# An attention and MLP kernel on one core: GpSimd takes over the split of one probability tile in three, the sign projections move one unit earlier, and the first MLP tiles are begun and activated while the last heads are still worked on

## The chip, the core and the metric

The kernel runs on one core of one Trainium2 chip. TensorE (PE in the rows) multiplies matrices into PSUM; ScalarE (ACT), VectorE (DVE) and GpSimd (POOL) work elementwise, GpSimd on SBUF alone; SyncE (SP) issues most transfers. The engines run side by side, each through its own instructions in order, and wait for one another by semaphores. The metric is the device time of a launch in microseconds.

## The reference

Attention over 2 batches of 8 heads, 768 tokens, head size 64, with a mask by hash bucket, then two MLPs over 1536 tokens with model size 512 and hidden size 2048.

```python
q_bits = (einsum('bhsd,dk->bhsk', q, proj) > 0)      # 6 bits: the bucket of a token
k_bits = (einsum('bhsd,dk->bhsk', k, proj) > 0)
mask = q_bucket[:, :, :, None] == k_bucket[:, :, None, :]
scores = where(mask, scale * q @ k.T, -1e9)
attn = exp(scores - max(scores)); attn = attn / (sum(attn) + 1e-9)
x = (attn @ v)                                        # 1536 x 512 over both batches
h = x @ w1_in;  x = where(h > 0, h, exp(min(h, 0)) - 1) @ w1_out
h = x @ w2_in;  out = (s * max(h, 0)**2 + b) @ w2_out
```

## The kernel before

Each product is made in the PE's reduced float format from a high part and a low part: every operand is split into `hi` (rounded) and `lo` (the rest), and a product takes the three terms hi·hi, hi·lo and lo·hi, or two where one side's parts are stacked.

**The heads.** Sixteen heads run as eight pairs. A pair is 12 units of 128 queries, six for each head; three units are a group (`HT = 3`), so a pair has four. Unit k runs on all engines with code written out by hand:

- PE (`unit`, L508 on): the scores of unit k+2 (four matmuls of 384 columns into `s_ps`, L440 and L441), the six transposes of the probabilities of unit k (L448), and then, by the place of k in its group: in the first unit the turn of a finished group (`turn`, L471), in the second and third one half each of the group's product with V (`times_v`, L461 and L462, six matmuls). The projection for the signs of the next head (`project`, L416 to L422, six matmuls) follows in units 1 and 7, the transposes of x (`transpose_x`, L429) in units 4 and 5. These two share the PSUM bank `prep_ps`.
- DVE (`unit`, L738 on): `keep_scores` of unit k+2 (L721), which frees `s_ps` for the next scores; in units 2, 3, 8 and 9 two `write_bits` (L714), one behind `keep_scores` and one behind `split_lo`; `split_lo` of unit k (L728); in the last unit of a group `invert` (L734, L736).
- ACT: the exponential of unit k+1 (L600), `keep_pv` and three copies that normalise a group, and `split_hi` of unit k; all its copies have line L595.
- GpSimd: the splits of q and k (L316 to L322), of V (L340, L342), of x (L329, L331) and of one weight tile in each pair (L349, L351).

The scores of a new head (made in units 4 and 10) need the bits of that head: three of the four `write_bits`. Scores n need `keep_scores` n-1.

**The MLP.** Each of two layers takes three chunks of 512 tokens, each chunk 16 hidden tiles: `hidden(f)` makes one in PSUM (L487, 12 matmuls of 512 columns), ACT applies two functions (L682, L685), DVE makes the result `g` (L802), its high part (L808) and its low part (L810), and `output(f)` multiplies it by the second weight (L505, 12 matmuls). There are four banks for hidden tiles (`HBANKS`) and three buffers for a split result (`GRING`). `hidden(f)` waits until L802 of tile f-4 has read its bank (`h_free`); L808 of tile j waits until `output(j-3)` has read its buffer (`g_free`). DVE takes L802, L808, L810 of one tile after another, in order. Output runs two tiles behind hidden. Chunk 0 of layer 1 needs the heads of batch 0 only, so `hidden(0)` to `hidden(3)` stand between the last units of the last pair. Weight tiles 0 to 7 (`wa`) are split during the heads, 8 to 15 (`wb`) after the last transpose of x, because one of the raw weight buffers holds x until then.

```python
pe.wait_ge(h_free, step + 1)                      # hidden: 4 given at the start, 1 by each L802
dve.wait_ge(g_free, step + 1)                     # L807: 3 given at the start, 1 by each output
nc.vector.tensor_copy(hi[:], g[:]).then_inc(g_made, 1)
```

## Time and profile before

| what | us |
|---|---|
| median of 3 runs (lowest, highest) | 846.91 (846.63, 848.03) |
| the profiled execution: its time, its span | 847.2, 845.4 |
| PE, DVE, ACT, POOL busy over the span | 94%, 51%, 40%, 26% |
| the heads, up to the first hidden tile | 0 to 304.6 |
| the rest of the heads with hidden tiles 0 to 3 | 304.6 to 328.8 |
| from the first output tile to the end | 328.8 to 845.4 |

The busy share is a mean over stages with different limits. In the page's 40 slices (21 us each) PE stands at 6 to 9 tenths over the heads, DVE at 7 and 8, and PE at 9 tenths in every slice from the seventeenth on but the last. The granted clock of PE is 6 tenths in the first slice, 8 in the second and 9 (90% or more) in all after it but the sixteenth. The time of a row is its start from the start of the span, then its duration; matmul rows overlap, since the end of one is modelled with its drain, so how long a step occupies PE is read from start to start. What stands in brackets is the idle time of the engine before the row and what ended it.

### The profile page before, as it was taken

To read this page: it belongs to the slowest core of one execution; us is meant where nothing else is said; L and a number is where in the kernel's file an instruction comes from. 1 tells how busy PE (TensorE), PEld (TensorE's weight loads), DVE (VectorE), ACT (ScalarE), POOL (GpSimd) and SP (SyncE) were. 2 spreads that over 40 slices of the span, in tenths; PEclk is the share of its full clock that TensorE was granted. 3 is DMA by queue.
4 is the path that set the end of the run, shared out by engine and by line. 5 is a ranking of instruction groups with operands and counts; after the bars stand their busy time and mean duration, and the time that the engine had idled before them with its cause. 6 is when DMAs were issued, how large, how long until landed. Compare 5 with 4: busy or idle time off the path is not lost.

```text
span 845.4 us, 11759 instructions
## 1 busy us (share of the span) xinstructions
PE 794.2 (94%) x3996; PEld 690.2 (82%) x3996; DVE 432.0 (51%) x734; ACT 337.2 (40%) x643; POOL 216.2 (26%) x182
## 2 busy tenths in 40 slices
PE   6798889889888997999999999999999999999998
PEld 5788888888788886888888888888888888888886
DVE  4788787878877845633433343334223433333223
ACT  4567676766767653222322232223222222212221
POOL 4226353452635124910000006666000000000000
PEclk6899999999999998999999999999999999999999
DMA  4333343233334102410000003222000100010001
GB/s 120 91 76 91 77 119 105 65 90 74 92 79 112 35 1 75 130 45 1 1 1 1 0 0 99 92 90 67 1 1 0 50 0 0 0 50 0 0 0 50
DMA packets 33255, 41.84 MB, mean 49 GB/s; under 512 B 3024, under 2 KB 21584, under 8 KB 33232
## 3 DMA queue, kind: packets, MB, share of 16 engines
q1 hardware_dynamic: 33008, 41.23, 17.3%
q10 hardware_dynamic: 224, 0.30, 0.2%
q8 instruction: 15, 0.25, 0.1%
q14 instruction: 8, 0.07, 0.0%
HBM read 26.58 MB, written 3.15 MB: 35 GB/s over the span
## 4 chain that ended last, share of the span: by engine, by line
PE 85%; DVE 7%; issue 5%; ACT 2%; DMA 0%; DVEq 0%; POOL 0%; SPq 0%; ACTq 0%
PE acc L505 31%; PE h_ps L487 31%; PE pt_ps L448 5%; PE s_ps L440 4%; PE pv_ps L461 3%; PE pv_ps L462 3%; PE s_ps L441 3%; DVE kt L714 2%; DVE pt_lo L728 1%; DVE probs L721 1%; DVE qt L714 1%; PE pv_ps L471 1%; ACT probs L600 1%; PE prep_ps L429 1%; PE prep_ps L422 1%
## 5 line engine op out<-in xcount | busy, mean ns | idle before, releaser
L682 ACT ACTIVATE r_sb<-h_ps 128x512 f32<-128x512 f32 x96 | 57.4, 598 | 359.0 <-PE h_ps L487 359.0
L728 DVE TENSOR_TENSOR pt_lo<-pt_ps,pt_hi 128x768 fp32r<-128x768 f32 x96 | 92.0, 958 | 39.2 <-ACT pt_hi L595 37.6
L804 DVE TENSOR_SCALAR g_sb<-e_sb,sb_scale 128x512 f32<-128x512 f32 x48 | 27.8, 578 | 158.3 <-ACT e_sb L685 158.3
L802 DVE SCALAR_TENSOR_TENSOR g_sb<-e_sb,h_ps 128x512 f32<-128x512 f32 x48 | 33.0, 687 | 147.3 <-ACT e_sb L685 147.3
L595 ACT ACTIVATE pt_hi<-pt_ps 128x768 fp32r<-128x768 f32 x96 | 77.9, 812 | 75.6 <-PE pt_ps L448 75.3
L721 DVE TENSOR_SCALAR_CACHE_REDUCE probs<-s_ps 128x768 f32<-128x768 f32 x96 | 91.9, 958 | 29.2 <-PE s_ps L441 26.0
L440 PE MATMUL s_ps<-kt,qt 128*128 128x384 f32 x192 | 72.3, 376 | 36.2 <-DVE qt L714 31.3
L600 ACT ACTIVATE probs<-probs,row_min 128x768 f32<-128x768 f32 x96 | 89.7, 934 | 11.3 <-DVE probs L721 11.1
L448 PE MATMUL pt_ps<-cst,probs 128*128 128x128 f32 x576 | 82.8, 282 | 0.0
L810 DVE TENSOR_TENSOR g_lo<-g_sb,g_hi 128x512 fp32r<-128x512 f32 x96 | 74.9, 780 | 3.3
L448 PEld LDWEIGHTS pt_ps<-cst,probs 128*128 128x128 f32 x576 | 72.2, 146 | 3.9
L487 PE MATMUL h_ps<-xt_hi,wa_hi 128*128 (+1 forms) x192 | 74.9, 390 | 0.1
L487 PE MATMUL h_ps<-xt_hi,wa_lo 128*128 (+1 forms) x192 | 74.8, 390 | 0.0
L487 PE MATMUL h_ps<-xt_hi,wb_lo 128*128 (+1 forms) x192 | 74.8, 389 | 0.0
L487 PE MATMUL h_ps<-xt_lo,wa_hi 128*128 (+1 forms) x192 | 74.8, 389 | 0.0
L487 PE MATMUL h_ps<-xt_lo,wb_hi 128*128 (+1 forms) x192 | 74.7, 389 | 0.0
L487 PE MATMUL h_ps<-xt_hi,wb_hi 128*128 (+1 forms) x192 | 74.7, 389 | 0.0
L461 PE MATMUL pv_ps<-pt_hi,v_nat 128*128 128x384 f32 x192 | 74.0, 386 | 0.0
L440 PEld LDWEIGHTS s_ps<-kt,qt 128*128 128x128 f32 x192 | 38.2, 199 | 41.8 <-DVE probs L721 28.0
L462 PE MATMUL pv_ps<-pt_lo,v_nat 128*128 128x384 f32 x192 | 67.9, 353 | 0.0
L441 PE MATMUL s_ps<-kt,qt 128*128 128x384 f32 x192 | 67.1, 349 | 0.0
L685 ACT ACTIVATE e_sb<-r_sb 128x512 f32<-128x512 f32 x96 | 60.7, 632 | 10.6
(87 smaller groups left out, 1538.8 us busy)
## 6 DMA issues: line engine op xcount, KB each, us to landing
qt<-kt SPq DMA_DIRECT2D x45, 192.0 KB, 2.7
w_raw<-w_in_dram SPq DMA_DIRECT2D x32, 256.0 KB, 2.8
w_raw<-w_out_dram SPq DMA_DIRECT2D x32, 256.0 KB, 2.9
raw<-qk_dram SPq DMA_DIRECT2D x15, 384.0 KB, 3.3
raw_v<-v_dram SPq DMA_DIRECT2D x16, 192.0 KB, 2.4
out_dram<-o_sb SPq DMA_DIRECT2D x12, 256.0 KB, 2.1
...
```

Of the source, the lines that this page charges most:

```text
L440: mm(s_ps[:, n, 0:HALF], q1, kt1[par][:, cols], start=True, stop=False)
L441: last = mm(s_ps[:, n, 0:HALF], q2, kt2[par][:, cols], start=False, stop=True)
L448: last = nc.tensor.transpose(pt_ps[k % 2][:, r * P:(r + 1) * P], probs[k % SRING][:, r * P:(r + 1) * P], ident)
L461: mm(pv_ps[:, 0:HALF], v_nat[par][:, kt, :], pt_hi[buf][:, kt, :], start=kt == 0, stop=False)
L462: last = mm(pv_ps[:, 0:HALF], v_nat[par][:, kt, :], pt_lo[buf][:, kt, :], start=False, stop=kt == TILES - 1)
L487: last = mm(bank[:], w[a][:, kt * P:(kt + 1) * P], x[b], start=n == 0, stop=n == 3 * KT - 1)
L505: last = mm(acc[n][:], lhs, rhs, start=f == 0 and j == 0, stop=f == FT - 1 and j == 2)
L595: return nc.scalar.activation(dst, src, ACT.Copy, scale=scale)
L600: nc.scalar.activation(probs[k % SRING][:], probs[k % SRING][:], ACT.Exp, bias=row_min[:, k:k + 1], scale=-1.0, accum_out=row_sum[:, k:k + ...
L721: ts(probs[k % SRING][:].rearrange("p (n c) -> p n c", n=2), s_ps[:, :, 0:HALF], CEILING, HUGE, ALU.min, ALU.min, accum_out=row_min[:, k:k ...
L728: tt(pt_lo[(k // HT) % 2][where], pt_ps[k % 2][:, 0:SEQ].rearrange("p (t c) -> p t c", t=TILES), pt_hi[(k // HT) % 2][where].bitcast(F32), ...
L810: tt(lo[:], g[:], hi[:].bitcast(F32), ALU.subtract).then_inc(g_ready, 1)
```

## The change

The rows of the order below name the instructions as the two programs list them, with the line of each program's own text.

The projection for the signs moves from units 1 and 7 to units 0 and 6, and the bits from units 2, 3, 8 and 9 to 1, 2, 7 and 8. On PE, in units 6 and 7 of a pair, before:

```order
L448 MATMUL pt_ps0<-cst,probs0 128x128 x6
L469 REGISTER_ALU
L471 MATMUL pv_ps<-cst,pv_sb 128x64 x3
L521 REGISTER_ALU
L83 REGISTER_ALU
L440 MATMUL s_ps<-kt1_1,qt1_1 128x384
L441 MATMUL s_ps<-kt2_1,qt2_1 128x384
L440 MATMUL s_ps<-kt1_1,qt1_1 128x384
L441 MATMUL s_ps<-kt2_1,qt2_1 128x384
L448 MATMUL pt_ps1<-cst,probs1 128x128 x6
```

and in the changed program:

```order
L474 MATMUL pt_ps0<-cst,probs0 128x128 x6
L498 MATMUL pv_ps<-cst,pv_sb 128x64 x3
L431 REGISTER_ALU
L436 MATMUL prep_ps<-kt1_0,planes_hi 128x384
L437 MATMUL prep_ps<-kt1_0,planes_lo 128x384
L436 MATMUL prep_ps<-kt1_0,planes_hi 128x384
L437 MATMUL prep_ps<-kt1_0,planes_lo 128x384
L442 MATMUL prep_ps<-kt2_0,planes_hi 128x384 x2
L548 REGISTER_ALU
L84 REGISTER_ALU
L460 MATMUL s_ps<-kt1_1,qt1_1 128x384
L461 MATMUL s_ps<-kt2_1,qt2_1 128x384
```

The six matmuls into `prep_ps` now stand behind the turn of unit 6 and ahead of the scores that unit 7 makes; before they stood behind that unit's product with V.

On DVE, units 6 to 8 in the changed program: L758 is `keep_scores`, L782 the normalising multiplication, L789 the low part of x, L751 `write_bits`, L765 `split_lo`:

```order
L789 TENSOR_TENSOR xt_lo<-prep_ps,xt_hi 128x384
L756 REGISTER_ALU
L758 TENSOR_SCALAR probs2,row_min<-s_ps 128x768
L84 REGISTER_ALU
L782 TENSOR_TENSOR w_raw1<-pv_ps,row_inv 128x3x64
L756 REGISTER_ALU
L758 TENSOR_SCALAR probs0,row_min<-s_ps 128x768
L740 REGISTER_ALU
L745 REGISTER_ALU
L751 TENSOR_SCALAR kt2_0<-prep_ps,cst 12x384
L763 ISA
L765 TENSOR_TENSOR pt_lo0<-pt_ps1,pt_hi0 128x6x128
```

Before, the first unit of a group had its `split_lo` too, and the normalising copies and x's high part were ACT's. Now GpSimd makes both parts of that tile (`split_pt`) from a copy that ACT writes to SBUF, and DVE normalises and makes the low part of x straight from PSUM.

On PE in chunk 0 of layer 1, at the place where bank `h_ps0` is taken by hidden tile 8 (the first with `wb`), before:

```order
L505 MATMUL acc3<-g_hi2,wa_hi 128x512
L505 MATMUL acc3<-g_lo2,wa_hi 128x512
L505 MATMUL acc3<-g_hi2,wa_lo 128x512
L487 MATMUL h_ps0<-xt_hi,wb_hi 128x512
L487 MATMUL h_ps0<-xt_lo,wb_hi 128x512
L487 MATMUL h_ps0<-xt_hi,wb_lo 128x512
```

and in the changed program:

```order
L532 MATMUL acc3<-g_hi0,wa_hi 128x512
L532 MATMUL acc3<-g_lo0,wa_hi 128x512
L532 MATMUL acc3<-g_hi0,wa_lo 128x512
L514 MATMUL h_ps0<-xt_hi,wb_hi 128x512
L514 MATMUL h_ps0<-xt_lo,wb_hi 128x512
L514 MATMUL h_ps0<-xt_hi,wb_lo 128x512
```

Before, output tile 5 (the sixth, in ring buffer 2) stood ahead of hidden tile 8; now it is output tile 0. The seven hidden tiles 0 to 6 are all made among the last steps of the heads, and outputs run seven tiles behind.

The diff, cut to what the prediction speaks of (the planes of signs are also loaded in a compact form of 48 columns and laid out by DVE; with that and the matmuls of `keep_warm` the start changes):

```diff
--- before.py
+++ after.py
-WARM = 12
+WARM, REWARM = 14, 5
 HBANKS, GRING = 4, 3
+BEGUN = HBANKS + GRING
...
-Z_UNIT = {1: 1, TILES + 1: 2}
-BITS_UNIT = {2: (1, (0, 1)), 3: (1, (2, 3)), TILES + 2: (2, (0, 1)), TILES + 3: (2, (2, 3))}
-X_UNIT = {4: 0, 5: 1}
+Z_UNIT = {0: 1, TILES: 2}
+BITS_UNIT = {1: (1, (0, 1)), 2: (1, (2, 3)), TILES + 1: (2, (0, 1)), TILES + 2: (2, (2, 3))}
+X_UNIT = {3: 0, 5: 1}
+X_LO_UNIT = {4: 0, 6: 1}
+W_PAIRS = EARLY // 2
...
 sync: pair
-                load_w(0, i, 0, i)
+                if w:
+                    load_w(0, i + 1, 0, i + 1)
...
 gpsimd
-            def split_x(i, n):
...
+            def split_pt(i, g):
+                G, buf = GROUPS * i + g, g % 2
+                pool.wait_ge(pt_kept, G + 1)
+                pool.nop(nofuse=True)
+                src = pt_raw[buf][:].rearrange("p (t c) -> p t c", t=TILES)
+                nc.gpsimd.tensor_copy(pt_hi[buf][:, :, 0:P], src).then_inc(pt_pool_hi, 1)
+                pool.wait_ge(pt_pool_hi, G + 1)
+                nc.gpsimd.tensor_tensor(pt_lo[buf][:, :, 0:P], src, pt_hi[buf][:, :, 0:P].bitcast(F32),
+                                        ALU.subtract).then_inc(pt_pool_done, 1)
...
-            def pair(i, first=False, more=True):
+            def pair(i, w=True, more=True):
+                split_pt(i, 0)
+                if w:
+                    split_w(at(wa_hi, i), at(wa_lo, i), i, 0, i + 1)
                 split_v(2 * i + 1, 1)
                 if more:
                     split_qk(2 * i + 2, 0)
-                if not first:
-                    split_x(i - 1, 0)
-                    split_x(i - 1, 1)
-                split_w(at(wa_hi, i), at(wa_lo, i), i, 0, i + 1)
+                split_pt(i, 1)
+                split_pt(i, 2)
                 if more:
                     split_v(2 * i + 2, 0)
                     split_qk(2 * i + 3, 1)
+                split_pt(i, 3)
...
 tensor: transpose_probs, times_v
-                wait(pe, pt_lo_done, u - 1)
+                G, t = GROUPS * i + (k - 2) // HT, (k - 2) % HT
+                if t == 0:
+                    wait(pe, pt_kept, G + 1)
+                else:
+                    wait(pe, pt_lo_done, 2 * G + t)
...
-                        pe.wait_ge(pt_lo_done, HT * G + HT)
+                        pe.wait_ge(pt_pool_done, G + 1)
+                        pe.wait_ge(pt_lo_done, 2 * G + 2)
...
 tensor: the start
-            for _ in range(WARM):
-                mm(pv_ps[:, 0:HALF], pt_hi[0][:, 0, 0:P], pt_hi[0][:, 0, :], start=True, stop=True)
+            keep_warm(WARM)
             project(0, 0)
+            keep_warm(REWARM)
...
             for k in range(AHEAD):
                 scores(k, k)
+                keep_warm(REWARM - 2)
...
 tensor: the end of the heads
             hidden(0, 0, 2)
             turn(PAIRS, -2)
             hidden(0, 0, 3)
             times_v(PAIRS, -1, range(TILES))
-            pe.wait_ge(x_kept, 2 * PAIRS - 2)
             transpose_x(PAIRS, 0)
+            hidden(0, 0, 4)
             turn(PAIRS, -1)
-            pe.wait_ge(x_kept, 2 * PAIRS - 1)
+            hidden(0, 0, 5)
+            pe.wait_ge(xt_lo_done, 2 * PAIRS - 1)
             transpose_x(PAIRS, 1)
-            def chunk(layer, c, begun=0):
+            hidden(0, 0, 6)
+            def chunk(layer, c, lead=2):
                 if layer:
                     pe.wait_ge(acc_free, KT * c + 2 * KT)
-                for f in range(FT + 1):
-                    if begun <= f < FT:
+                for f in range(FT + lead):
+                    if f < FT and (lead == 2 or f >= lead):
                         hidden(layer, c, f)
-                    if f >= 2:
-                        output(layer, c, f - 2)
-                output(layer, c, FT - 1)
-            chunk(0, 0, HBANKS)
+                    if f >= lead:
+                        output(layer, c, f - lead)
+            chunk(0, 0, BEGUN)
...
 scalar
+                if t == 0:
+                    wait(act, pt_pool_done, G - 1)
+                    copy(pt_raw[(k // HT) % 2][:], src).then_inc(pt_kept, 1)
+                else:
+                    copy(pt_hi[(k // HT) % 2][:, :, t * P:(t + 1) * P],
+                         src.rearrange("p (t c) -> p t c", t=TILES)).then_inc(pt_hi_done, 1)
...
-            def normalise(i, g):
...
-                copy(x_raw[n][:], prep_ps[:, 0:HALF]).then_inc(x_kept, 1)
+                copy(xt_hi[:, x_cols(i, n)], prep_ps[:, 0:HALF]).then_inc(xt_hi_done, 1)
...
 scalar: the end of the heads
+            activate(0, 0, 0)
             keep_pv(PAIRS, -2)
-            normalise(PAIRS, -2)
+            activate(0, 0, 1)
+            activate(0, 0, 2)
             keep_pv(PAIRS, -1)
-            keep_x(PAIRS - 1, 0)
-            normalise(PAIRS, -1)
-            keep_x(PAIRS - 1, 1)
+            x_hi(PAIRS - 1, 0)
+            activate(0, 0, 3)
+            x_hi(PAIRS - 1, 1)
+            for f in range(HBANKS, FT):
+                activate(0, 0, f)
...
 vector
+            def normalise(i, g):
...
+                tt(x_nat[:, (g % 2) * HT:(g % 2 + 1) * HT, par * DH:(par + 1) * DH],
+                   pv_ps[:, 0:HT * DH].rearrange("p (t d) -> p t d", t=HT),
+                   row_inv[:, c].unsqueeze(2).to_broadcast([P, HT, DH]), ALU.mult).then_inc(x_done, 1)
+            def x_lo(i, n):
+                dve.wait_ge(xt_hi_done, 2 * i + n + 1)
+                cols = x_cols(i, n)
+                tt(xt_lo[:, cols], prep_ps[:, 0:HALF], xt_hi[:, cols].bitcast(F32), ALU.subtract).then_inc(xt_lo_done, 1)
...
 vector: unit
+                if third == 1 and not (first and k < 2 * HT):
+                    normalise(i, k // HT - 2)
+                if k in X_LO_UNIT and not first:
+                    x_lo(i - 1, X_LO_UNIT[k])
                 if k < UNITS - AHEAD or more:
                     keep_scores(u + AHEAD, (k + AHEAD) % UNITS)
...
-                split_lo(u, k)
+                if third:
+                    split_lo(i, k)
...
 vector: the end of the heads (split_g holds the three operations of lines 802 to 810 with their waits)
-            dve.wait_ge(x_kept, 2 * PAIRS)
+            split_g(0, 0, 0)
+            normalise(PAIRS, -2)
+            split_g(0, 0, 1)
+            split_g(0, 0, 2)
+            x_lo(PAIRS - 1, 0)
+            normalise(PAIRS, -1)
+            x_lo(PAIRS - 1, 1)
+            dve.wait_ge(xt_lo_done, 2 * PAIRS)
             dve.nop().then_inc(acc_free, KT)
+            for f in range(GRING, FT):
+                split_g(0, 0, f)
```

## Rows read from the trace of the kernel before

**Rows 1.** Windows of core 0: busy time of each engine, then PEclk, DMA share, GB/s

```profile
100.84:136.59 35.75, 31.40 (x212) 30.00 (x211) 29.10 (x53) 25.91 (x55) 16.40 (x17) 1.00 0.36 92
136.59:173.91 37.32, 32.98 (x212) 31.51 (x211) 29.09 (x53) 25.91 (x55) 16.39 (x16) 0.95 0.34 88
```

**Rows 2.** Waits of the whole run: us in total, times, longest

```profile
PE s_ps L440 <- DVE qt L714: 31.3, 16, 4.3
```

**Rows 3.** Timeline of PE in one pair: start, duration, instruction, idle before

```profile
149.40 0.88 PE L471 MATMUL pv_ps<-cst,pv_sb 128*128 128x64 f32 x6 [0.51 <-ACT pv_sb L595]
150.09 0.42 PE L440 MATMUL s_ps<-kt,qt 128*128 128x384 f32 x1
...
153.65 0.34 PE L440 MATMUL s_ps<-kt,qt 128*128 128x384 f32 x1
...
156.07 0.34 PE L440 MATMUL s_ps<-kt,qt 128*128 128x384 f32 x1
...
157.42 0.83 PE L471 MATMUL pv_ps<-cst,pv_sb 128*128 128x64 f32 x6
159.99 0.44 PE L440 MATMUL s_ps<-kt,qt 128*128 128x384 f32 x1 [1.74 <-DVE qt L714]
```

**Rows 4.** Timeline of DVE in the same pair, units 8 and 9

```profile
154.55 0.96 DVE L721 TENSOR_SCALAR_CACHE_REDUCE probs<-s_ps 128x768 f32<-128x768 f32 x1 [0.76 <-PE s_ps L441]
...
156.20 0.96 DVE L728 TENSOR_TENSOR pt_lo<-pt_ps,pt_hi 128x768 fp32r<-128x768 f32 x1
...
157.84 0.16 DVE L734 SCALAR_TENSOR_TENSOR row_inv<-row_sum,cst 128x3 f32<-128x3 f32 x1
...
158.25 0.96 DVE L721 TENSOR_SCALAR_CACHE_REDUCE probs<-s_ps 128x768 f32<-128x768 f32 x1
```

**Rows 5.** Timeline of PE at both ends of the heads and at the first outputs

```profile
16.48 0.66 PE L440 MATMUL s_ps<-kt,qt 128*128 128x384 f32 x1 [1.15 <-DVE probs L721]
...
55.03 0.34 PE L440 MATMUL s_ps<-kt,qt 128*128 128x384 f32 x1
...
276.71 0.34 PE L440 MATMUL s_ps<-kt,qt 128*128 128x384 f32 x1
...
304.60 0.47 PE L487 MATMUL h_ps<-xt_hi,wa_hi 128*128 128x512 f32 x1
...
324.53 0.52 PE L429 MATMUL prep_ps<-cst,w_raw 128*128 128x128 f32 x3 [0.96 <-ACT w_raw L595]
328.77 0.80 PE L505 MATMUL acc<-g_hi,wa_hi 128*128 128x512 f32 x1 [3.72 <-DVE g_lo L810]
...
336.01 0.39 PE L487 MATMUL h_ps<-xt_hi,wa_hi 128*128 128x512 f32 x1
```

**Rows 6.** Timeline of DVE at the first results g

```profile
327.56 0.43 DVE L808 CAST g_hi<-g_sb 128x512 fp32r<-128x512 f32 x1
...
328.63 0.68 DVE L802 SCALAR_TENSOR_TENSOR g_sb<-e_sb,h_ps 128x512 f32<-128x512 f32 x1
...
331.12 0.55 DVE L808 CAST g_hi<-g_sb 128x512 fp32r<-128x512 f32 x1
331.71 2.78 DVE L810 TENSOR_TENSOR g_lo<-g_sb,g_hi 128x512 fp32r<-128x512 f32 x1
...
357.35 0.43 DVE L808 CAST g_hi<-g_sb 128x512 fp32r<-128x512 f32 x1
357.81 1.41 DVE L810 TENSOR_TENSOR g_lo<-g_sb,g_hi 128x512 fp32r<-128x512 f32 x1
```

**Rows 7.** Timeline of POOL, first split of a `wb` tile and last

```profile
330.24 1.15 POOL L349 CAST wb_hi<-w_raw 128x1024 f32 x1 [2.96 <-DMA w_raw<-w_out_dram]
...
358.84 2.64 POOL L351 TENSOR_TENSOR wb_lo<-w_raw,wb_hi 128x1024 f32 x1 [0.16 <-POOL wb_hi L349]
```

**Rows 8.** Group by line, POOL over the heads: count, busy us, mean ns, idle before

```profile
L322 POOL TENSOR_TENSOR kt<-raw,kt 128x768 fp32r<-128x768 f32 x15 | 27.5, 1830 | 1.3
```

**Rows 9.** Timeline of DVE in the first pair, `invert`

```profile
27.09 1.60 DVE L734 SCALAR_TENSOR_TENSOR row_inv<-row_sum,cst 128x3 f32<-128x3 f32 x1
```

More of the change, by code:

```diff
@@ L9 @@
 F32R = mybir.dt.float32r
-BF16 = mybir.dt.bfloat16
 ACT = mybir.ActivationFunctionType
@@ L66, in laid_planes @@
 def laid_planes(proj):
[L69 to L76 removed]
+    c = np.zeros((P, 2, 2, 2, BITS), np.float32)
+    for side, rows in ((0, slice(DH, P)), (1, slice(0, DH))):
+        for n, sign in ((0, -1), (1, 1)):
+            c[rows, 0, side, n] = proj
+            c[rows, 1, side, n] = sign
+    return c.reshape(P, 8 * BITS)
 def wait(eng, sem, value):
@@ L282, in _ @@
             pair(0)
-            with sp.Fori(1, PAIRS - 2) as i:
+            with sp.Fori(1, W_PAIRS) as i:
                 pair(i)
-            pair(PAIRS - 2, after=False)
-            pair(PAIRS - 1, nxt=False, after=False)
+            with sp.Fori(W_PAIRS, PAIRS - 2) as i:
+                pair(i, w=False)
+            pair(PAIRS - 2, w=False, after=False)
+            pair(PAIRS - 1, w=False, nxt=False, after=False)
+            for f in range(W_PAIRS + 1, EARLY):
+                load_w(0, f, 0, f)
             sp.wait_ge(xt_pe, 2 * PAIRS)
@@ L632, in unit @@
                 first = isinstance(i, int) and i == 0
-                if third == 1 and not (first and k < 2 * HT):
-                    normalise(i, k // HT - 2)
                 if k < UNITS - 1 or more:
@@ new lines, in next_hi @@
+            def next_hi(c):
+                for n in range(KT):
+                    if n < KT - 1:
+                        act.wait_ge(acc_done, c * (KT - 1) + n + 1)
+                    else:
+                        act.wait_ge(g_free, c * FT + GRING + FT)
+                    cols = n * TOKENS + c * CHUNK if isinstance(c, int) else None
+                    where = slice(cols, cols + CHUNK) if isinstance(c, int) else bass.ds(c * CHUNK + n * TOKENS, CHUNK)
+                    copy(xt_hi[:, where], acc[n][:]).then_inc(acc_hi_done, 1)
@@ L696, in _ @@
+            x_hi(PAIRS - 1, 0)
[3 more added lines that the diff above has]
+                activate(0, 0, f)
+            next_hi(0)
+            with act.Fori(1, CHUNKS) as c:
+                for f in range(FT):
+                    activate(0, c, f)
+                next_hi(c)
+            with act.Fori(0, CHUNKS) as c:
+                for f in range(FT):
+                    activate(1, c, f)
         @block.vector
@@ L777, in _ @@
             dve.wait_ge(consts_in, 16)
-            for block in range(4):
+            for block in (2, 0, 1, 3):
                 write_bits(0, 0, block)
@@ L826, in x_cols @@
+            with dve.Fori(0, CHUNKS) as c:
+                for f in range(FT):
+                    split_g(1, c, f)
+                keep_output(c)
 def x_cols(i, n):
```

231 lines of the change are left out of this document (114 added, 117 removed).

## The prediction

> **What bounds the kernel now.** I read the windows first, then the waits, then the timeline of PE beside that of DVE. The MLP (from 328.8 us on) is bound by PE, whose matmuls stand back to back there, so it can lose time and not win any. What can be won lies in the heads and at their end. A pair of heads takes 35.75 us where PE keeps its full clock and 37.32 us where the granted clock averages 0.95 [rows 1]; the mean of pairs 1 to 6 is (276.71 - 55.03) / 6 = 36.95 us [rows 5]. The waits give the cause: PE sat idle 31.3 us in 16 waits for the sign bits that DVE writes [rows 2], one in each half of a pair, 1.74 us each [rows 3]. At the end of the heads PE idles again: 3.72 us before the first output, for `g_lo` [rows 5].
>
> PE's own work in a pair: a unit with a product takes 156.07 - 153.65 = 2.42, unit 7 with its projection 153.65 - 150.09 = 3.56, so the projection is 1.06 (0.08 of the rest is a first matmul); scores and transposes of a unit with a turn take 157.42 - 156.07 = 1.35 and the turn 150.09 - 149.40 = 0.69 [rows 3]. Sum: 8 x 2.42 + 4 x 2.04 + 2 x 1.06 + 0.9 for the transposes of x and first matmuls = 30.5. The other 5.2 of the 35.75 are waits.
>
> **The heads, step by step.** DVE in units 8 and 9: `keep_scores` and a `write_bits` together 156.20 - 154.55 = 1.65, `split_lo` and the next `write_bits` 157.84 - 156.20 = 1.64, `invert` 0.41, a `keep_scores` alone 0.96 + 0.08 = 1.04 [rows 4].
> - Removed from DVE: four `split_lo` in a pair, 4 x 0.99 = 4.0. Added: four multiplications of 192 columns and two subtractions of 384. Between nothing and the 0.96 of a full tile each [rows 4]; by columns I take 0.4 and 0.6, so 2.8. DVE does 1.2 less in a pair.
> - The projection moves ahead of the scores of the next unit. This removes the wait for bits (they are written five products earlier than needed) but not the queue on DVE: `keep_scores` of that unit now waits until PE has done the projection and the scores, though bits could be written meanwhile. From there DVE has, in order, two times (1.65 + 1.64), `invert`, `keep_scores`: 6.58 + 0.41 + 1.04 = 8.0. Scores of the next head need that last `keep_scores`.
>   In the second half of a pair: scores of unit 7 start at 0, are read from 0.9, DVE is through at 8.9 to 9.0. PE has 2.42 + 2.42 + 2.04 = 6.9 until it wants them. So 2.1 is waited. In the first half the transposes of x (0.3) move into this stretch: 1.8. A third wait, for `pv_sb` in unit 6 (0.51 before [rows 3]), becomes 0.7, as ACT has x ahead of it.
>   A pair at full clock: 30.5 + 2.1 + 1.8 + 0.7 = 35.1, against 35.75.
> - Three copies of ACT for each group go (ACT's 25.9 of 35.75 us [rows 1]): they bounded nothing.
> - GpSimd has 16.4 busy in a pair [rows 1]. The splits of probabilities add at most two operations of 1.83 [rows 8] four times, 14.6; x's splits and half of the weight tiles go. It stays under 31 of 35. Queued behind a split are those of V, q and k: the split of group 0 is done about 5 us into the pair, V's follows its product (end of unit 2), q and k of the next head end near 14, their projection comes at 17. Products with V want group g's part four units after it was kept, some 10 us, and it is there in 3 to 7. Hidden; uncovered, each us late would cost one.
> - The clock falls after such waits in part of the cases: (36.95 - 35.75) = 1.2 a pair. The new waits are as long, so I leave 1.3. Pairs 1 to 6: 36.4 instead of 36.95, gain 3 (from 0, if DVE's chain is 0.5 longer, to 11, if no clock is lost). Pair 7 up to the first hidden tile: 27.9 before [rows 5], 27.1 by the same count: 0.8.
> - The start: pair 0 takes 55.03 - 16.48 = 38.6 [rows 5]; with its projection a unit earlier it should take what others do, less the products it lacks: 34.5, gain 4. The first scores come earlier through smaller planes and the extra matmuls keep the clock: 3, between 0 and 4.
> Heads together: 11 less, bounds 3 and 20.
>
> **The end of the heads.** From the first hidden tile to hidden tile 4 before: 336.01 - 304.60 = 31.4 [rows 5], for 4 hidden and 2 output tiles (6 x 2.72), two units' transposes and products (3.4), two turns, one whole product (2.1), two transposes of x (0.6), together 23.9. So 7.5 are waits and half clock (1.8 of it: the two outputs from 328.77 took 7.24 instead of 5.44). The change fills all of that: by the order of the diff hidden tiles 4, 5 and 6 stand where PE waited, and their banks are read in time (result 0 about 8 us before hidden tile 4 wants its bank, result 3 about 0.6 us before hidden tile 7 does). Gain 7.5.
>
> But it adds a wait that stands in no row. With outputs seven tiles behind, PE comes to hidden(f), f = 8 to 15, having just finished output(f-8). Its bank is freed by L802 of tile f-4. Behind it on DVE in order is nothing, ahead of it stands L808 of tile f-5, which waits for a buffer that output(f-8) frees. So each time PE finishes an output, DVE must do L808 and L810 of one tile and L802 of the next, before PE may go on; nothing else is queued on PE. Cost of one: signal 0.2, L808 and L810 328.63 - 327.56 = 1.07, L802 0.68, signal 0.06: 2.0 [rows 6]. While GpSimd splits weight tiles, L808 and L810 take longer: six pairs, from 331.12 (3.4 with the wait in L810) to 357.35 (1.87), mean 3.0 [rows 6]; a wait is then 3.9. GpSimd splits from 330.24 to 361.48, that is from 5.7 after the last transpose begins, for 31 us [rows 5, 7]. In the changed order (0 is the start of hidden tile 2) that is 21 to 52, and the waits begin at 23, 33, 42, 52: four at 3.9, four at 2.0, 23.6 in all.
> The clock: after 3.72 idle it cost 1.8, so 4 x 1.8 = 7.2; after 1.74 idle twice in a pair 1.2, so 0.6 for each of the other four, 2.4. Together 33. Lower bound 8 x 2.0 = 16, upper 8 x 3.9 + 8 x 1.8 = 46. Less the 7.5: the end costs 25.5 more, bounds 8.5 and 38.
>
> From output tile 8 on nothing differs. Sum: 847.2 (profiled; the span is 845.4, and 846.9 is the median) - 11 + 25 = 861; I say 860.
>
> **The rivals.**
> - PE becomes the bound of the heads. For it: DVE does 1.2 less, and DVE is the engine waited for. Against: the chain of 8.0 holds neither of the removed `split_lo` at its place. A pair would take 32.5: 6 x 4.4 + 2 + 7 = 35 less, and with the end's 25 more 837. This is the case on the other side; it decides if DVE's chain from the scores of unit 7 is under 6.
> - The waits at the ring are there but bare: no half clock, no blocking. For it: the clock holds through many waits of 1.74. Against: the 3.72. End +8.5, heads -11: 844.5.
> - GpSimd stands in DVE's way in the heads. `invert` has once taken 1.60, when GpSimd's subtraction of k ran [rows 9]; otherwise 0.16 [rows 4]. GpSimd's share of a pair grows from 16 to about 27. With 1.4 more in each of the two chains of a pair, 2.8 x 7 = 20: 880. The Trainium skill (SBUF — State Buffer, Who interferes with whom) says that a DVE instruction with two SBUF inputs is held for the whole of a GpSimd instruction that reads SBUF. The trace agrees with 1.60 in one of 32; by my count of times the chain's `invert` meets the end of a short operation, so I give this little.
> - The change does not do what it says in the heads (the wait for bits stays): then it gains 7, and the end decides: 865, inside the forecast.
>
> **How the numbers follow.** Forecast 0.68 (its own range 850 to 870), PE bound 0.10, bare ring 0.12, GpSimd in the way 0.10. The range 844 to 871 leaves out the first rival, the last and a little of the second's lower side. Under 0.2% (1.7 us) a measurement of this kernel tells nothing: faster 0.10 + 0.08 of the second = 0.18, same 0.06, slower 0.76.
>
> **What would show it.** Right: idle of PE before hidden tiles 8 to 15 of the first chunk, released by L802's successor, eight times 2 to 4 us; no wait for bits; a wait for `keep_scores` in units 4 and 10 of 1 to 2 us; no idle between hidden tile 2 and output 0; the first hidden tile near 293. Wrong: PE back to back in chunk 0, a pair under 34 or over 37.5, or a first hidden tile after 302.

## The result, and the profile after

| | before | after |
|---|---|---|
| median (lowest to highest), us | 847.39 (846.63 to 848.03) | 859.12 (855.59 to 863.72) |
| ratio, 95% interval | | 1.014 (1.009 to 1.019) |
| the profiled execution: its time, its span | 847.2, 845.4 | 863.7, 861.9 |
| first hidden tile | 304.60 | 295.67 |
| from there to the end | 540.8 | 566.2 |

The change makes the kernel slower by 1.4%, as forecast (860). The profiled executions differ by 16.5: the heads give 8.9 back, what follows costs 25.4. The executions of the changed kernel spread over 8 us, those of before over 1.4, and the profiled one is the longest; by the medians the loss is 11.7.

The page of the changed kernel, busy shares and slices (PE 94% before, DVE 51%, ACT 40%, POOL 26%):

```profile
PE 803.1 (93%) x4009; PEld 690.9 (80%) x4009; DVE 416.5 (48%) x752; ACT 318.1 (37%) x547; POOL 274.5 (32%) x214
PE   7888898889998996788999999999999999999998
PEclk9999999999999998799999999999999999999999
```

The shares moved as the edit moved work, from DVE and ACT to GpSimd, and say nothing of the loss. The slices do: PE's slices at 6 and 7 tenths are the sixteenth and seventeenth (323 to 366 us), and there the clock stands at 8 and 7 tenths too.

The waits of the changed kernel, PE as the waiting engine, with DVE's largest wait on PE beside them (us in total, times, longest):

```profile
PE s_ps L460 <- DVE probs L758: 26.9, 33, 2.3
PE h_ps L514 <- DVE g_sb L866: 21.2, 8, 4.1
DVE g_hi L872 <- PE acc L532: 66.0, 13, 8.5
```

The wait for bits [rows 2], 31.3 us in 16, is gone but for one of 1.3 us at the very start. In its place stand two: one for `keep_scores`, and the new one of hidden tiles for their bank. The third line is its mirror: DVE waits for PE as well, though PE waits for DVE. In this stretch each waits for the other in turn.

PE's timeline of the changed kernel, at hidden tile 0 and at the first four hidden tiles that waited (start, duration, instruction, idle before):

```profile
295.67 0.47 PE L514 MATMUL h_ps<-xt_hi,wa_hi 128*128 128x512 f32 x1 [0.49 <-issue]
...
331.96 0.50 PE L514 MATMUL h_ps<-xt_hi,wb_hi 128*128 128x512 f32 x1 [3.86 <-DVE g_sb L866]
...
343.45 0.79 PE L514 MATMUL h_ps<-xt_hi,wb_hi 128*128 128x512 f32 x1 [4.13 <-DVE g_sb L866]
...
354.78 0.79 PE L514 MATMUL h_ps<-xt_hi,wb_hi 128*128 128x512 f32 x1 [4.04 <-DVE g_sb L866]
...
365.01 0.50 PE L514 MATMUL h_ps<-xt_hi,wb_hi 128*128 128x512 f32 x1 [1.84 <-DVE g_sb L866]
```

Hidden tiles 8, 9 and 10 wait some 4 us, 11 to 15 wait 1.84 each: 12.0 + 9.2 = 21.2. The duration 0.79 against 0.50 marks the matmuls that start at half clock behind two of the long waits.

DVE of the changed kernel at the second wait and at the fourth:

```profile
339.35 0.67 DVE L872 CAST g_hi<-g_sb 128x512 fp32r<-128x512 f32 x1 [7.44 <-PE acc L532]
...
363.20 0.43 DVE L872 CAST g_hi<-g_sb 128x512 fp32r<-128x512 f32 x1 [8.47 <-PE acc L532]
363.66 0.69 DVE L874 TENSOR_TENSOR g_lo<-g_sb,g_hi 128x512 fp32r<-128x512 f32 x1
364.27 0.68 DVE L866 SCALAR_TENSOR_TENSOR g_sb<-e_sb,h_ps 128x512 f32<-128x512 f32 x1
```

DVE sits idle 8.47 us until PE has finished an output, then does the cast, the low part and the next result, and releases PE at the end of the third: 364.27 + 0.68 + 0.06 = 365.01. The 0.2 + 1.07 + 0.68 + 0.06 of the forecast is 1.84 here. The cast at 339.35 belongs to the 4.13: there the three take 0.71, 2.66 and 0.68, up to 343.40.

GpSimd of the changed kernel, the second tile it splits in this stretch and the last:

```profile
328.33 2.44 POOL L361 TENSOR_TENSOR wb_lo<-w_raw,wb_hi 128x1024 f32 x1 [0.17 <-POOL wb_hi L359]
...
351.25 2.34 POOL L361 TENSOR_TENSOR wb_lo<-w_raw,wb_hi 128x1024 f32 x1 [0.16 <-POOL wb_hi L359]
```

The last split ends at 353.6. The three long waits end before 355, the five short ones come after it. I had counted the splits to run until 52 us past the start of hidden tile 2 (304.63) and to stretch a fourth wait; they ended at 49.0, and the fourth wait began only at 58.5. I had put the waits some 9.7 apart. They begin 11.2 to 12.4 apart, because the clock lost behind each also pushes the next one back.

The windows, PE, PEld, DVE, ACT and POOL busy us with instructions, then the granted clock: an early pair, a later one at full clock, the one behind it, and the whole stretch from the first hidden tile to the end, of the changed kernel:

```profile
79.75:117.01 37.26, 33.37 (x210) 31.45 (x210) 27.91 (x55) 23.67 (x43) 23.84 (x21) 0.95 0.34 88
154.25:189.47 35.22, 31.77 (x211) 29.84 (x211) 27.52 (x55) 23.66 (x43) 20.55 (x19) 1.00 0.31 78
189.47:226.27 36.80, 33.35 (x210) 31.38 (x211) 27.56 (x55) 23.65 (x43) 20.54 (x19) 0.95 0.30 75
295.67:861.90 566.23, 541.74 (x2358) 445.68 (x2358) 196.10 (x321) 128.00 (x212) 93.55 (x54) 0.98 0.09 30
```

and the same stretch of the kernel before:

```profile
304.60:845.40 540.80, 532.56 (x2358) 441.24 (x2358) 198.63 (x317) 131.42 (x222) 89.14 (x52) 0.99 0.09 29
```

The two stretches hold the same 2358 matmuls, so the rows split the 25.4 exactly: PE idle is 566.23 - 541.74 = 24.5 against 8.2, 16.3 more, and the same matmuls take 541.74 - 532.56 = 9.2 longer, which is the clock.

The pair at full clock takes 35.22, where 35.75 stood [rows 1] and 35.1 was forecast; where GpSimd still splits a weight tile, in the first four pairs, a pair is some 0.4 longer (37.26 against 36.80, both at a mean granted clock of 0.95).

### The profile page after: what moved, and what is told of

Read it like the earlier page. It is cut to its first block, busy times and chain, and to the rows that moved or that the text cites. A ratio compares the mean times of both kernels' runs of the same rounds, so it can differ in the third digit from the quotient of the medians.

```text
span 861.9 us, 11790 instructions
## 1 busy us (share of the span) xinstructions
PE 803.1 (93%) x4009; PEld 690.9 (80%) x4009; DVE 416.5 (48%) x752; ACT 318.1 (37%) x547; POOL 274.5 (32%) x214
## 4 chain that ended last, share of the span: by engine, by line
PE 81%; DVE 11%; issue 5%; ACT 1%; DVEq 0%; DMA 0%; ACTq 0%; SPq 0%
PE h_ps L514 32%; PE acc L532 30%; PE pt_ps L474 4%; PE s_ps L460 3%; PE s_ps L461 3%; PE pv_ps L488 2%; PE pv_ps L489 2%; DVE probs L758 2%; DVE pt_lo L765 2%; DVE kt L751 2%; PE pv_ps L498 2%; DVE qt L751 2%; DVE g_lo L874 1%; PE prep_ps L436 1%; ACT probs L634 1%
## 5 line engine op out<-in xcount | busy, mean ns | idle before, releaser
L758 DVE TENSOR_SCALAR_CACHE_REDUCE probs<-s_ps 128x768 f32<-128x768 f32 x96 | 91.9, 957 | 39.1 <-PE s_ps L461 35.8
L514 PE MATMUL h_ps<-xt_hi,wb_hi 128*128 (+1 forms) x192 | 79.1, 412 | 21.2 <-DVE g_sb L866 21.2
L460 PE MATMUL s_ps<-kt,qt 128*128 128x384 f32 x192 | 69.7, 363 | 28.2 <-DVE probs L758 26.9
L514 PE MATMUL h_ps<-xt_lo,wb_hi 128*128 (+1 forms) x192 | 78.2, 407 | 0.0
L514 PE MATMUL h_ps<-xt_hi,wb_lo 128*128 (+1 forms) x192 | 78.1, 407 | 0.0
L629 ACT ACTIVATE pt_hi<-pt_ps 128x768 fp32r<-128x768 f32 x64 | 52.0, 812 | 66.5 <-PE pt_ps L474 66.5
L872 DVE CAST g_hi<-g_sb 128x512 fp32r<-128x512 f32 x96 | 42.8, 446 | 69.0 <-PE acc L532 66.0
L359 POOL CAST wa_hi<-w_raw 128x1024 f32 (+1 forms) x16 | 17.5, 1094 | 183.8 <-PE acc L532 180.3
L765 DVE TENSOR_TENSOR pt_lo<-pt_ps,pt_hi 128x768 fp32r<-128x768 f32 x64 | 61.3, 958 | 28.3 <-ACT pt_hi L629 27.3
L874 DVE TENSOR_TENSOR g_lo<-g_sb,g_hi 128x512 fp32r<-128x512 f32 x96 | 72.6, 756 | 3.3
```

The lines of the kernel that those rows point to most:

```text
L460: mm(s_ps[:, n, 0:HALF], q1, kt1[par][:, cols], start=True, stop=False)
L514: last = mm(bank[:], w[a][:, kt * P:(kt + 1) * P], x[b], start=n == 0, stop=n == 3 * KT - 1)
L758: ts(probs[k % SRING][:].rearrange("p (n c) -> p n c", n=2), s_ps[:, :, 0:HALF], CEILING, HUGE, ALU.min, ALU.min, accum_out=row_min[:, k:k ...
L765: tt(pt_lo[(k // HT) % 2][where], pt_ps[k % 2][:, 0:SEQ].rearrange("p (t c) -> p t c", t=TILES), pt_hi[(k // HT) % 2][where].bitcast(F32), ...
L874: tt(lo[:], g[:], hi[:].bitcast(F32), ALU.subtract).then_inc(g_ready, 1)
```

## The experiments

Each is a small edit of the changed kernel or of the one before. Ratios are against the kernel before (846.7 to 847.2 in these comparisons).

| experiment | median us | ratio (95%) | first hidden tile | from there to the end |
|---|---|---|---|---|
| outputs six behind | 827.19 | 0.976 (0.974 to 0.978) | 292.56 | 533.5 |
| four buffers for results | 827.66 | 0.977 (0.975 to 0.979) | 292.30 | 533.5 |
| before, outputs seven behind | 875.90 | 1.035 (1.033 to 1.037) | 303.95 | 569.8 |
| weight splits as memsets | 849.37 | 1.004 (1.002 to 1.005) | 289.54 | 557.2 |
| outputs two behind, hidden tiles 4 to 6 not begun early | 830.77 | 0.980 (0.978 to 0.982) | 294.91 | 536.2 |
| before, signs a unit earlier | 842.32 | 0.993 (0.991 to 0.995) | 299.44 | 540.9 |
| six behind, signs at their old units | 831.49 | 0.983 (0.981 to 0.986) | 296.37 | 533.5 |
| six behind, no filler matmuls at the start | 831.18 | 0.981 (0.979 to 0.984) | 295.89 | 533.7 |
| six behind, bits ahead of `keep_scores` | 814.16 | 0.963 (0.961 to 0.965) | 278.32 | 533.5 |
| the same, and `invert` a unit later | 806.19 | 0.952 (0.950 to 0.954) | 271.06 | 533.5 |

### The wait at the ring

My theory: outputs stand seven tiles behind, and seven is the number of PSUM banks (4) plus that of result buffers (3), so at hidden(f) every bank and every buffer is full and PE can go on only through DVE. The rival: with the low part slowed by GpSimd, DVE is simply too slow in this stretch, whatever the depth. One tile less of lead tells them apart, and so does one buffer more.

```diff
-            def chunk(layer, c, lead=2):
+            def chunk(layer, c, lead=2, begun=0):
...
-                    if f < FT and (lead == 2 or f >= lead):
+                    if begun <= f < FT:
...
-            chunk(0, 0, BEGUN)
+            chunk(0, 0, BEGUN - 1, BEGUN)
```

> The changed kernel with one edit: in chunk 0 of layer 1 outputs run six tiles behind hidden tiles, not seven (output 0 stands ahead of hidden tile 7). Ring theory: the buffer that L872 wants is freed a hidden and an output tile (5.4 us) before PE wants the bank, against a chain of 2 to 4 us on DVE, so all eight waits go (21.2 us idle in the profile) and with them the half clock behind them (5 to 12 us): 826 to 831 us, against 859. Rival, the waits come from GpSimd's weight splits and move with them: some of the three waits of 4 us stay, 838 to 845. Rival, PE would only wait for its weight tiles (wb) instead: 840 to 850.

Seven hidden tiles are still begun among the heads, but outputs follow six behind. DVE's timeline with outputs six behind:

```profile
322.33 2.25 DVE L872 CAST g_hi<-g_sb 128x512 fp32r<-128x512 f32 x1 [3.56 <-PE acc L532]
...
350.17 2.79 DVE L874 TENSOR_TENSOR g_lo<-g_sb,g_hi 128x512 fp32r<-128x512 f32 x1
```

and its windows, the first 130 us of the MLP and the whole of it:

```profile
290.00:420.00 130.00, 129.49 (x599) 108.36 (x598) 61.65 (x86) 35.76 (x62) 39.89 (x23) 1.00 0.16 49
292.56:826.10 533.54, 530.22 (x2358) 439.64 (x2358) 200.32 (x321) 128.33 (x212) 94.91 (x54) 1.00 0.10 32
```

DVE's operations are slowed as much as before, up to 2.79 us, and PE doesn't wait once: its idle time in these 130 us is the 0.5 ahead of the first hidden tile. The rival falls. The whole stretch takes 533.5 where the changed kernel takes 566.2: 21.2 less idle and 541.74 - 530.22 = 11.5 less for the same matmuls. This 32.7 is the price of the ring waits with their clock, and I had summed 33.

```diff
-HBANKS, GRING = 4, 3
-BEGUN = HBANKS + GRING
+HBANKS, GRING = 4, 4
+BEGUN = 7
...
-            for f in range(GRING, FT):
+            for f in range(3, FT):
```

> The changed kernel with four buffers for split results in place of three, outputs still seven tiles behind. Ring theory: L872 of tile f-5 then wants output f-9, done 5.4 us before PE comes to hidden tile f, so the eight waits go as with six tiles behind: 826 to 831 us, within 2 us of that kernel. Rival, the order with seven tiles is itself at fault (banks, weights or the late outputs), the ring is not: 850 to 860.

The same from the other side: outputs still seven behind, one more buffer, 827.66. It isn't the depth as such that costs, but depth equal to banks plus buffers.

The converse, the kernel before with outputs of its first chunk seven behind:

```diff
-            def chunk(layer, c, begun=0):
+            def chunk(layer, c, begun=0, lead=2):
...
-                for f in range(FT + 1):
+                for f in range(FT + lead):
...
-                    if f >= 2:
-                        output(layer, c, f - 2)
-                output(layer, c, FT - 1)
+                    if f >= lead:
+                        output(layer, c, f - lead)
...
-            chunk(0, 0, HBANKS)
+            chunk(0, 0, HBANKS, 7)
```

> The kernel before with one edit: hidden tiles 4, 5 and 6 of chunk 0 stand ahead of output 0, and outputs of that chunk run seven tiles behind. Heads and their end are as before. Ring theory: the same eight waits appear and cost 26 to 33 us with the clock; hidden tile 4 still waits for the first result (the 3.7 us stay), nothing is won: 870 to 881 us. Rival, the waits of the changed kernel need its new work on DVE and GpSimd: 845 to 852.

Its PE waits:

```profile
PE s_ps L440 <- DVE qt L713: 31.1, 16, 4.3
PE h_ps L487 <- DVE g_sb L801: 20.8, 9, 3.6
...
326.94 0.79 PE L487 MATMUL h_ps<-xt_hi,wa_hi 128*128 128x512 f32 x1 [2.53 <-DVE g_sb L801]
```

The last line is hidden tile 4, which waits for the first result: 2.53, where output 0 waited 3.72 before. The other eight are hidden tiles 8 to 15 at the ring, 20.8 - 2.5 = 18.2 us (3.6, 3.1 and six of 1.93), in a kernel that has nothing else of the change, and 875.9 - 846.75 = 29.2 us on the median. The heads are as they were (31.1 for bits). So the ring wait needs no other part of the change.

### GpSimd's part in the wait

Three waits are 4.0 and five 1.84. My theory: DVE's two operations on a result are slowed while GpSimd splits weights. The rival: the first three wait for something else of the first tiles, the end of the heads' work on DVE or ACT. In this kernel GpSimd writes the `wb` tiles of the first layer by two memsets, so it reads nothing. The weights of hidden tiles 8 to 15 of that layer are zero here: the kernel leaves their part of layer 1 out. Its loop over these tiles on GpSimd is also written out.

```diff
+            def blank_w(hi, lo, count, buf, landed):
+                pool.wait_ge(w_landed[buf], 32 * landed)
...
+                nc.gpsimd.memset(hi.bitcast(F32), 0.0).then_inc(w_hi, 1)
+                pool.wait_ge(w_hi, count + 1)
+                nc.gpsimd.memset(lo.bitcast(F32), 0.0).then_inc(w_split, 1)
...
-                    split_w(at(wb_hi, 2 * j + n), at(wb_lo, 2 * j + n), EARLY + 2 * j + n, 1 - n,
+                    blank_w(at(wb_hi, 2 * j + n), at(wb_lo, 2 * j + n), EARLY + 2 * j + n, 1 - n,
```

> The changed kernel, with the splits of weight tiles 8 to 15 of layer 1 on GpSimd replaced by two memsets of the same tiles (these weights are zero then, so layer 1 leaves them out). GpSimd then only writes there. Theory that its reads hold up L874 and L872: the three waits of 4 us become 1.8 to 2.0 like the other five, and less clock is lost: 6 us fewer in idle and 1 to 5 in clock, 847 to 853. Rival, writes hold DVE up as well (or another cause, such as the transfers, makes them long): 857 to 861.

The waits of this kernel, and its first wait at the ring:

```profile
PE h_ps L522 <- DVE g_sb L874: 14.7, 8, 1.8
...
323.81 0.50 PE L522 MATMUL h_ps<-xt_hi,wb_hi 128*128 128x512 f32 x1 [1.84 <-DVE g_sb L874]
```

All eight are 1.84, the first three too: 6.5 us less idle. DVE of this kernel beside a memset of GpSimd:

```profile
331.17 0.43 DVE L880 CAST g_hi<-g_sb 128x512 fp32r<-128x512 f32 x1 [7.42 <-PE acc L540]
331.63 0.69 DVE L882 TENSOR_TENSOR g_lo<-g_sb,g_hi 128x512 fp32r<-128x512 f32 x1
```

and GpSimd at the same time:

```profile
331.27 1.22 POOL L367 MEMSET wb_hi<- 128x1024 f32 x1 [0.56 <-DMA w_raw<-w_out_dram]
332.55 0.95 POOL L369 MEMSET wb_lo<- 128x1024 f32 x1
```

The low part takes its bare 0.69 beside a GpSimd instruction that only writes, and 2.7 beside one that reads. The Trainium skill (SBUF — State Buffer, Who interferes with whom) says just this: a DVE instruction with two SBUF inputs collides with a GpSimd instruction that reads SBUF, not with one that only writes it. The trace agrees. It also shows the other direction: the memset that began during DVE's cast took 1.22 instead of 0.95.

The stretch to the end is 9.0 shorter than the changed kernel's (566.2 - 557.2), for 6.5 less idle. Against the 533.5 without ring waits it is 23.7 longer: 14.7 of idle and 9.0 of clock, 1.1 for each short wait. Of the changed kernel's 11.5 of clock that leaves 11.5 - 5 x 1.1 = 6.0 for the three long waits, 2.0 each. These are means: behind a short wait the next one follows after 7.6 us or after 9.2, against 5.44 + 1.84 = 7.3 for two tiles and a wait, so a single one costs 0.3 or 1.9, and the 1.6 between them is what a fall of the clock costs in the heads too.

### What beginning early is worth by itself

Hidden tiles 4 to 6 out of the heads, and outputs two behind as before; what stays is that ACT and DVE turn tiles 0 to 3 into results while the last products run.

```diff
-            hidden(0, 0, 4)
...
-            hidden(0, 0, 5)
...
-            hidden(0, 0, 6)
...
-            chunk(0, 0, BEGUN)
+            chunk(0, 0, 2, HBANKS)
```

> The changed kernel with its depth undone: hidden tiles 0 to 3 begun among the heads and outputs two tiles behind as before, but the early activations on ACT and DVE kept. Theory: without depth there are no ring waits, and since results 0 to 2 are ready early, PE waits at the end of the heads only for the last turn and transpose (up to 2 us, and the 3.7 us before output 0 are gone): 828 to 832, at most 3 us more than with six tiles behind. Rival, depth is what fills the end of the heads: 833 to 836.

PE's waits at the end of the heads in this kernel:

```profile
312.87 0.88 PE L498 MATMUL pv_ps<-cst,pv_sb 128*128 128x64 f32 x6 [0.25 <-ACT pv_sb L626]
...
314.36 0.52 PE L449 MATMUL prep_ps<-cst,w_raw 128*128 128x128 f32 x3 [0.61 <-DVE w_raw L779]
...
316.20 0.47 PE L532 MATMUL acc<-g_hi,wa_hi 128*128 128x512 f32 x1 [1.32 <-DVEq L897]
```

The 3.72 before the first output [rows 5] is down to 1.32, and the 1.32 are no longer for a result: L897 is the instruction by which DVE frees the accumulators behind the last low part of x. The stretch takes 536.2: 4.6 less than before, and 2.7 more than with seven tiles begun and outputs six behind (533.5); on the medians it is 3.6, where I had expected at most 3. Of the 7.5 that I gave to the filling, 4.6 come from the earlier results and 2.7 from tiles 4 to 6; together 7.3.

### The heads: the move, the relief, the start

The kernel before with the signs a unit earlier, and nothing else:

```diff
-Z_UNIT = {1: 1, TILES + 1: 2}
-BITS_UNIT = {2: (1, (0, 1)), 3: (1, (2, 3)), TILES + 2: (2, (0, 1)), TILES + 3: (2, (2, 3))}
+Z_UNIT = {0: 1, TILES: 2}
+BITS_UNIT = {1: (1, (0, 1)), 2: (1, (2, 3)), TILES + 1: (2, (0, 1)), TILES + 2: (2, (2, 3))}
...
-                    if k > TILES and not first:
+                    if k >= TILES and not first:
```

> The kernel before with the move alone: projection in units 0 and 6, bits in units 1, 2, 7 and 8. GpSimd, ACT and DVE keep their work, the end is untouched. Theory of the prediction: the move makes the gain of the heads and DVE's relief makes next to none, as the chain of 8.0 holds none of the removed instructions: pairs near 36.4 and 4 us in pair 0: 838 to 843. Rival, the move is only good with DVE relieved (it has a split_lo in units 0 and 3 as well): 846 to 852.

And the converse, six behind with the signs and x back at their old units, so that of the two edits to the heads only the relief by GpSimd is left (smaller planes and filler matmuls stay, the bits go back to units 2, 3, 8 and 9, and the edit of the lead is the one above):

```diff
-Z_UNIT = {0: 1, TILES: 2}
...
-X_UNIT = {3: 0, 5: 1}
-X_LO_UNIT = {4: 0, 6: 1}
+Z_UNIT = {1: 1, TILES + 1: 2}
...
+X_UNIT = {4: 0, 6: 1}
+X_LO_UNIT = {5: 0, 7: 1}
```

> The changed kernel with outputs six tiles behind (827.2 us), and the projection and bits back in units 1, 7 and 2, 3, 8, 9 (the transposes of x go to units 4 and 6). GpSimd's splits and DVE's relief stay. Theory of the prediction: the wait for bits is back in each half and the relief buys little: pairs of 36.5 to 37.5, pair 0 with its long wait: 831 to 838. Rival, the relief is what shortens the heads: 824 to 829.

The wait for bits in this second kernel:

```profile
PE s_ps L460 <- DVE qt L751: 28.6, 15, 3.2
```

It is back almost in full, with two of three `split_lo` left on DVE. To leave the start out, count from the scores made in unit 10 of pair 0 to the first hidden tile. The windows, in this order: before, relief alone, move alone, both (six behind):

```profile
50.08:304.60 254.52, 225.87 (x1465) 216.63 (x1465) 201.51 (x361) 179.41 (x376) 107.93 (x105) 0.97 0.33 83
42.62:296.37 253.75, 225.07 (x1464) 216.29 (x1465) 191.08 (x375) 164.12 (x295) 154.21 (x130) 0.97 0.31 77
51.26:299.44 248.18, 222.75 (x1464) 210.61 (x1465) 200.37 (x360) 182.47 (x375) 108.04 (x105) 0.99 0.33 85
44.01:292.56 248.55, 224.31 (x1465) 211.32 (x1465) 191.13 (x374) 165.56 (x295) 153.87 (x130) 0.99 0.31 79
```

In the changed kernel's own trace the stretch takes 295.67 - 44.14 = 251.5. Here the relief brings 0.7 and the move 6.3. But only half of the 6.3 is waiting: PE idles 28.65 before and 25.43 with the move, and the other half is that the same matmuls take less. Of the seven parts of this stretch (six pairs and the rest) the clock fell in five before, in five with the relief alone, in two with the move alone, in two with both and in four in the changed kernel. Three falls fewer at 1.6 are 4.8 of the 6.3, which leaves the move 1.5 by itself, some 0.2 in a pair (35.38 to 35.45 at full clock, where 35.44 and 35.74 stood). How many pairs are met differs between executions too, so the move's share is surer from the medians: 846.74 - 842.32 = 4.4 by itself, 831.49 - 827.19 = 4.3 on top of the relief. What is shown is that the move shortens PE's waits (1.74 us become 1.44) and that the clock then falls less often, and that taking work from DVE does next to nothing in this stretch. That DVE's order is what bounds a pair follows from the last two experiments below.

Ahead of this stretch it is the other way round. The move alone reaches the scores of unit 10 at 51.26 against 50.08 before, and with the relief at 44.01 against 42.62 without the move. In pair 0 the wait for bits of 4.34 us in unit 4 only turns into one of 3.59 for `keep_scores`.

The start, six behind without the filler matmuls that keep the clock:

```diff
-WARM, REWARM = 14, 5
+WARM = 12
...
-            keep_warm(REWARM)
...
-                keep_warm(REWARM - 2)
```

> The changed kernel with outputs six tiles behind (827.2 us), without the matmuls of keep_warm behind the first projection and the first scores, and with 12 at the start as before. Theory: PE falls to half clock in the first 20 us as before, which makes scores and transposes of the first units longer; of the 3 us taken for the start about 2 are the clock's: 828 to 832. Rival, the first units are bound by DVE and ACT whatever the clock: 826 to 828.

Its window from 10 to 20 us:

```profile
10.00:20.00 10.00, 7.79 (x27) 6.71 (x26) 2.89 (x6) 3.79 (x7) 4.57 (x5) 0.52 0.56 152
```

and with them (six behind):

```profile
10.00:20.00 10.00, 8.16 (x49) 6.98 (x48) 5.78 (x12) 5.73 (x11) 7.12 (x6) 1.00 0.69 177
```

In the same 10 us PE is about as busy, but at a granted clock of 0.52 it gets 27 matmuls done and at 1.00 it gets 49, of which 6 are filler. The scores made in unit 4 come at 28.84 and at 25.33: the filler is worth 3.5 us at the start, 3.3 at the first hidden tile and 4.0 on the median.

### Shortening the chain of 8.0

The forecast says that the pair is bound by what DVE does between the scores of one unit and the `keep_scores` two units on, and that bits could be written while `keep_scores` waits. If that is right, the same instructions in another order must be faster. First, both blocks of bits of units 1 and 7 go ahead of `keep_scores`:

```diff
+                if blocks and third == 1:
+                    write_bits(2 * i + off, off % 2, blocks[0])
+                    write_bits(2 * i + off, off % 2, blocks[1])
+                    blocks = ()
```

> The changed kernel with outputs six tiles behind (827.2 us) and one more edit: in units 1 and 7 DVE writes both blocks of bits ahead of keep_scores, in the time in which it waits for the projection and the scores of that unit. Chain theory: two blocks (1.3) start 0.7 before the scores can be read, so the chain from there to the keep_scores that PE wants shrinks by about 0.7 in each half of a pair, 15 times 0.7 = 10 us, and up to 5 of clock: 812 to 818. Rival, the wait of PE in units 4 and 10 has another cause than DVE's order (the transposes, ACT): 825 to 829. Rival, keep_scores comes later and delays the exponential and with it the transposes: slower than 829.

Then `invert` also moves behind the next unit's `keep_scores`:

```diff
-                if third == 2:
-                    invert(i, k // HT)
+                if third == 0 and not (first and k == 0):
+                    invert(i, k // HT - 1)
+                if not more and k == UNITS - 1:
+                    invert(i, GROUPS - 1)
```

> The kernel with bits first, and invert of a group moved behind the keep_scores of the next unit, so that the 0.4 us (and what GpSimd adds to it) leave the chain. Chain theory: another 15 x 0.4 = 6 us off: 805 to 813, and PE waits under 0.5 us in units 4 and 10. Rival, once the chain is short PE is bound by its own matmuls and by the wait for pv_sb in unit 6: within 2 us of the kernel with bits first.

PE's waits with bits ahead alone, in units 4 and 10:

```profile
126.88 0.45 PE L460 MATMUL s_ps<-kt,qt 128*128 128x384 f32 x1 [0.80 <-DVE probs L758]
...
144.42 0.45 PE L460 MATMUL s_ps<-kt,qt 128*128 128x384 f32 x1 [1.01 <-DVE probs L758]
```

PE's waits in units 10 and 4 of the last kernel, and the window of a pair:

```profile
140.56 0.44 PE L460 MATMUL s_ps<-kt,qt 128*128 128x384 f32 x1 [0.60 <-DVE probs L758]
...
156.64 0.44 PE L460 MATMUL s_ps<-kt,qt 128*128 128x384 f32 x1 [0.37 <-DVE probs L758]
...
123.43:156.64 33.21, 31.56 (x211) 29.77 (x211) 27.39 (x55) 23.46 (x43) 20.74 (x19) 1.00 0.39 99
```

DVE is as busy as in a pair of the changed kernel (27.39 against 27.52), PE too (31.56 and 31.77), and the pair takes 33.21 instead of 35.22 at the same full clock. The wait in unit 10 goes from 1.44 over 1.01 to 0.60, that in unit 4 from 1.27 (0.85 in the later pairs) over 0.80 to 0.37. I had expected both under 0.5. The granted clock is 1.00 over the whole run in all four executions of this kernel. With bits ahead alone it is 1.00 in two of the four, the profiled one among them, and 0.998 and 0.994 in the others, which took 814.65 and 816.74 us.

This version, 806.19 us (805.41 to 806.38), beats both kernels: 4.8% under the kernel before, 6% under the changed one.

## Why the prediction was right

- **The ring.** Forecast: hidden tiles 8 to 15 wait for the result of tile f-4, 4 x 3.9 + 4 x 2.0 = 23.6. Measured: 12.0 + 5 x 1.84 = 21.2. The mechanism is shown from both sides (six behind, a fourth buffer) and in the kernel before. Mis-sized: three waits met GpSimd's splits where four were counted. The splits ended 3 us sooner and the waits stand further apart (11.2 to 12.4 us, not 9.7); either would have spared the fourth.
- **The clock behind it.** Forecast 9.6 (1.8 behind a long wait, 0.6 behind a short one), measured 11.5 (2.0 and 1.1). The 0.6 came from waits that stand twice in a pair; these follow each other after 7.6 to 9.2 us. That the sum is right, 32.7 against 33, is partly luck: the wait was put 2.4 too high and its clock 1.9 too low.
- **What is filled.** Forecast 7.5, measured 540.8 - 533.5 = 7.3. No idle of PE stood between hidden tile 2 and output 0.
- **The pair.** Forecast 35.1 at full clock, measured 35.22 (35.61 in a pair with a weight split). The chain of 8.0, in units 7 to 10 of the changed kernel's DVE:

```profile
146.18 0.96 DVE L758 TENSOR_SCALAR_CACHE_REDUCE probs<-s_ps 128x768 f32<-128x768 f32 x1 [1.30 <-PE s_ps L461]
...
152.74 0.24 DVE L771 SCALAR_TENSOR_TENSOR row_inv<-row_sum,cst 128x3 f32<-128x3 f32 x1
153.23 0.96 DVE L758 TENSOR_SCALAR_CACHE_REDUCE probs<-s_ps 128x768 f32<-128x768 f32 x1
```

and PE at its end:

```profile
154.25 0.44 PE L460 MATMUL s_ps<-kt,qt 128*128 128x384 f32 x1 [1.44 <-DVE probs L758]
```

  From 146.18 to 153.23 + 0.96 = 154.19 are 8.0, and PE is released 0.06 later. The wait is 1.44 where 2.1 was forecast, since PE reaches this place 0.7 later than counted. In the first half it is 1.27 here and 0.85 in the later pairs (forecast 1.8). The pair comes out right nonetheless, as the length of the chain sets it and not PE's own work: what PE needs more it waits less.
- **The heads' sum.** Forecast 11, measured 8.9 in the profiled execution. The start brings 50.08 - 44.14 = 5.9 of the 7, the pairs behind it 3.0 of the 3.8. In the start the mechanism was wrong and the size right by luck: 4 of the 7 were to come from the earlier projection in pair 0, and the move alone makes that part 1.2 longer. The filler matmuls brought 3.5; the rest must lie with the smaller planes and the relief, which no run here separates. The pairs are where executions differ: with the same instructions in the heads, the first hidden tile came at 295.67, 292.56, 292.30 and 289.54. A pair is 35.22 or some 36.8, by whether the clock fell in it, and I gave one number for all. On the best of them the gain is 15, on the profiled one 8.9.
- **The rivals.** PE as the bound of the heads (837) fell: PE waits 26.9 us for `keep_scores`. The bare ring (844.5) fell on 11.5 us of clock and on GpSimd's part. GpSimd in the way of `invert` (880) is real and small: 0.58 to 0.60 instead of 0.16 in three of the pairs, at most 0.45 each, and 0.56 and 0.83 at the end of the heads. The windows of pairs with a fallen clock give 37.26 and 37.24 early in the heads, where those stretched ones stand, and 36.80 and 36.82 later. With bits ahead of `keep_scores` the same three take 0.38, 0.20 and 0.18, with GpSimd's work unchanged, and the pairs 34.22, 34.06 and 34.03, later 34.01. Both fit it; no run here takes that contention alone away. GpSimd's own share of a pair was put at 27 and is 20.5 to 23.8.
- **The total.** 863.7 in the profiled execution where 861 was summed, 859.1 as the median where 860 was forecast. With executions from 855.6 to 863.7, a hit within 1 us is luck; the terms of the sum are right to 2.4 us each.

What stays open: why a fall of the clock meets one pair and spares the next with equal waits. The traces show that it costs 1.6 a pair when it comes. It came in four of the changed kernel's seven parts, where such waits are up to 1.44, and in none of the profiled execution with waits of 0.80 and 1.01. Two other executions of that kernel have a granted clock of 0.998 and 0.994, and nothing shows where it fell in them.
